# A linear-attention and mixture-of-experts kernel: block 0's x in halves, and another order in the drain behind the last block

## The chip, the cores and the metric

The kernel runs on one core of a Trainium2 chip, in one launch. Its time is the device time of an execution in microseconds (us). Engines are named as in the profile: PE is TensorE (matmuls), PEld its weight loads, DVE is VectorE, ACT is ScalarE, POOL is GpSimd, SP is SyncE, which here only issues DMAs.

## What is computed

```
phi(x): a = S1 x, b = S2 x (8 values each); phi = outer(a, b), 64 values
kv = phi(k)^T v,  z = sum phi(k);   attn = phi(q) kv / (phi(q) z + 1e-6)        # 4 batches, 4 heads, 1088 tokens, dim 32
x  = attn as 4352 tokens x 128
xn = x / sqrt(mean(x*x) + 1e-6) * rms_g
y  = (silu(xn w_gate) * (xn w_val)) w_out                                        # hidden size 1536
logits = y phi2                                                                  # 32 slots, 4 for each of 8 experts
D = softmax of logits over tokens (each slot);  slot_input = D^T y               # 32 x 128
slot_out[e] = relu(slot_input[e] w1[e]) w2[e]                                    # hidden size 1024, 8 experts
C = softmax of logits over slots (each token);  out = C slot_out                 # 4352 x 128
```

All inputs and outputs are float32. The three large products of the second layer are made from a rounded high part and a low part of each operand (`xh`, `xl`, `wgh`, `wgl`, ...), with three matmuls for each product.

## The kernel before

The program is written engine by engine; every engine has its own list of instructions in program order, and semaphores join them. The order is by hand, there is no planner.

**Blocks.** The tokens are split into nine blocks: 0 to 7 of 512 tokens (two for each batch) and block 8 (`NB`) of the 256 tokens that remain. A block is run by `whole_block` in 12 steps `c`, one for each 128 hidden columns: `gate_value` (6 matmuls of 512 columns, L1012), then SiLU on ACT, product `hid` on DVE (L764), rounding `hh` on ACT (L527), rest `hl` on DVE (L770), and `output` (3 matmuls, L1025). The gate matmuls run `LAG` = 3 steps ahead of the output matmuls. Between these steps the attention and the normalisation of the next block are made.

**The head.** Before block 0 there is no earlier block to hide behind. Its x goes through `attention` (DVE, L715), `squares` (ACT, L492), `mean_square` (DVE, L722 and L724), `inverse_rms` (POOL, L424), `normalised` (DVE, L731), `normalised_T` (PE, L981, into `bank_a`), `scaled_T` (ACT, L496, `xh`) and `split_x` (DVE, L737, `xl`). Among these ACT rounds thirds of the three weight matrices (`split_hi`, L568) and POOL forms what rounding leaves (`split_lo`, L419). Piece x of matrix n is n = 0 gate, 1 val, 2 out. In program order ACT has val 0, out 0, val 1, squares, out 1 and so on, and POOL has gate 0, gate 1, val 0, out 0, val 1, `inverse_rms(0)`. `keep_clock(n)` is n matmuls of the identity with itself whose result nobody reads. SP and ACT issue the input loads; ACT's list has the last 64 keys of every batch (`k_rem`, rows of 256 bytes, L474).

**The drain.** A product of slots needs the maximum over all tokens of each slot's logit. `cmax_a` is the maximum over blocks 0 to 6 (28 tiles of 128 tokens, `NA`); in block 8 their logits get that maximum subtracted (L836), and ACT takes the exponential afterwards (L595). Behind block 8, PE makes its logits, DVE the maximum over the last six tiles (L865, L868), PE transposes it, DVE reduces it (`cm_all`, L870), PE spreads it, DVE subtracts it (L875), ACT takes the exponential (L600). `dispatch` sums exp(logit) x y in four groups of 32 partitions, the first 28 tiles in one bank, the last six in another. ACT rescales the first (`part_a`, L606), DVE adds them (L879), PE sums the four groups (`rep`), DVE divides (L882 to L886), PE transposes (L1161), ACT copies (`slotT`, L609). Then come the experts: `hidden` in four calls of 4 matmuls (n is the half of the experts, hf the half of the 1024 columns), Relu on ACT (L618), four transposes for each call (`hidden_T`, L1175), copies of each expert's own rows into the zeroed `hTz` (DVE, L893), and `slots_out`. Last, `s_out` is copied (L621), spread by `rep` and copied (`so4`, L623), and nine groups of output matmuls with the transposed combine weights `combT` follow; DVE and ACT scale them (L907, L628), SP stores them (L395, L399).

## Time and profile before

| | |
|---|---|
| time, median of 3 runs | 309.48 us (308.49 to 310.48) |
| the profiled execution | 311.83 us |
| its span, first to last instruction | 309.7 us |
| mean granted TensorE clock | 0.981 of full |
| PE busy | 295.4 us (95%), 2599 matmul instructions |
| PEld, DVE, ACT, POOL busy | 240.7, 224.2, 165.9, 29.7 us |
| chain that ended last | PE 87%, DMA 4%, DVE 3%, SP's queue 2%; its largest line, L915 (matmuls), 82% |

The table says how full the engines are over the whole span. The chain follows the work back from the last instruction to what released each piece, so it says which of that work set the end. The granted clock has two levels, 1.00 (2.4 GHz) and 0.50 (1.2 GHz); a stretch with a number between them has both.

### The profile page before, as it was taken

The numbers are of one execution on the slowest core, as the hardware profiler recorded it, in microseconds if no ns is written. First come the engines' busy times: TensorE is split into PE (matmuls) and PEld (weight loads), VectorE is DVE, ScalarE is ACT, GpSimd is POOL, SyncE is SP. The second block draws the span as 40 slices with busy tenths as digits, with TensorE's granted clock in tenths as the row PEclk, the third lists the DMA queues.
The fourth block names the chain that finished last, engine by engine and source line by source line (L and its number), as shares of the span: only waits on it lengthen the run. The fifth ranks groups of instructions, "written<-read, shape, count | busy, mean of one in ns | idle before, by whom it ended". The sixth has DMA issues, their size and how long they took to land.

```text
span 309.7 us, 6608 instructions
## 1 busy us (share of the span) xinstructions
PE 295.4 (95%) x2599; PEld 240.7 (78%) x2599; DVE 224.2 (72%) x438; ACT 165.9 (54%) x313; POOL 29.7 (10%) x49
## 2 busy tenths in 40 slices
PE   7769999999999999999999999999999999998985
PEld 7668788888888888888888778887888788896363
DVE  4733979786789688959877797687678758875144
ACT  1643566634755557355665564466545555557412
POOL 1356001000100010002500100020010001000000
PEclk9997999999999999999999999999999999999995
DMA  7999200000001200100030013999100100110007
GB/s 186 354 228 203 70 3 1 2 0 2 0 11 25 71 0 11 28 1 2 13 69 23 0 17 69 418 358 271 26 3 0 25 11 0 17 21 0 4 4 286
DMA packets 34864, 21.94 MB, mean 71 GB/s; under 512 B 19473, under 2 KB 31506, under 8 KB 34834
## 3 DMA queue, kind: packets, MB, share of 16 engines
q1 hardware_dynamic: 34162, 21.13, 24.9%
q10 hardware_dynamic: 672, 0.39, 0.6%
q8 instruction: 20, 0.33, 0.4%
q14 instruction: 10, 0.08, 0.1%
HBM read 17.45 MB, written 2.23 MB: 64 GB/s over the span
## 4 chain that ended last, share of the span: by engine, by line
PE 87%; DMA 4%; DVE 3%; SPq 2%; issue 1%; POOL 1%; ACT 1%; DVEq 0%; ACTq 0%; POOLq 0%
PE bank L915 82%; DMA area<-in_moe_w_out 4%; PE bank L954 2%; PE bank L981 1%; SPq L333 1%; PE bank L1175 1%; POOL wol L419 0%; DVE hid L764 0%; POOL wvl L419 0%; DVE area L907 0%; DVE cmax_a L821 0%; POOL rstd L424 0%; DVE hl L770 0%; SPq L339 0%; DVE area L731 0%
## 5 line engine op out<-in xcount | busy, mean ns | idle before, releaser
L764 DVE TENSOR_TENSOR hid<-bank,silu 128x512 f32<-128x512 f32 (+1 forms) x108 | 71.0, 657 | 49.9 <-PE bank L915 27.0
L519 ACT ACTIVATE silu<-bank 128x512 f32<-128x512 f32 (+1 forms) x108 | 61.9, 573 | 69.5 <-PE bank L915 68.5
L770 DVE TENSOR_TENSOR hl<-hid,hh 128x512 fp32r<-128x512 f32 (+1 forms) x108 | 70.2, 650 | 0.1
L527 ACT ACTIVATE hh<-hid 128x512 fp32r<-128x512 f32 (+1 forms) x108 | 64.9, 601 | 3.5 <-DVE hid L764 3.5
L915 PE MATMUL bank<-hh,woh 128*128 128x512 f32 (+1 forms) x108 | 43.4, 402 | 0.4 <-DVE hl L770 0.4
L915 PE MATMUL bank<-xh,wgh 128*128 128x512 f32 (+1 forms) x108 | 43.1, 399 | 0.5 <-DVE hid L764 0.5
L915 PE MATMUL bank<-xh,wgl 128*128 128x512 f32 (+1 forms) x108 | 41.3, 382 | 0.0
L915 PE MATMUL bank<-xh,wvh 128*128 128x512 f32 (+1 forms) x108 | 41.3, 382 | 0.0
L915 PE MATMUL bank<-xh,wvl 128*128 128x512 f32 (+1 forms) x108 | 41.1, 380 | 0.0
L915 PE MATMUL bank<-hh,wol 128*128 128x512 f32 (+1 forms) x108 | 41.1, 380 | 0.0
L915 PE MATMUL bank<-xl,wgh 128*128 128x512 f32 (+1 forms) x108 | 41.1, 380 | 0.0
L915 PE MATMUL bank<-hl,woh 128*128 128x512 f32 (+1 forms) x108 | 40.9, 379 | 0.0
L915 PE MATMUL bank<-xl,wvh 128*128 128x512 f32 (+1 forms) x108 | 40.8, 378 | 0.0
L424 POOL TENSOR_TENSOR rstd<-msq,mhalf 128x4 f32<-128x4 f32 (+1 forms) x9 | 8.8, 976 | 192.0 <-DVE msq L724 191.9
L915 PEld LDWEIGHTS bank<-hh,woh 128*128 128x128 f32 x108 | 20.3, 188 | 5.0 <-DVE hl L770 0.6
L915 PEld LDWEIGHTS bank<-xh,wgh 128*128 128x128 f32 x108 | 20.5, 189 | 4.3 <-DVE hid L764 0.9
L915 PEld LDWEIGHTS bank<-xl,wvh 128*128 128x128 f32 x108 | 20.4, 189 | 4.1
L915 PEld LDWEIGHTS bank<-xh,wgl 128*128 128x128 f32 x108 | 20.4, 189 | 4.1
L915 PEld LDWEIGHTS bank<-xh,wvl 128*128 128x128 f32 x108 | 20.3, 188 | 4.1
L915 PEld LDWEIGHTS bank<-hh,wol 128*128 128x128 f32 x108 | 20.3, 188 | 4.1
L915 PEld LDWEIGHTS bank<-xh,wvh 128*128 128x128 f32 x108 | 20.4, 189 | 3.9
L915 PEld LDWEIGHTS bank<-xl,wgh 128*128 128x128 f32 x108 | 20.5, 190 | 3.5
(134 smaller groups left out, 352.1 us busy)
## 6 DMA issues: line engine op xcount, KB each, us to landing
area<-in_moe_w SPq DMA_DIRECT2D x1, 4096.0 KB, 12.7
area<-in_moe_w SPq DMA_DIRECT2D x8, 512.0 KB, 7.0
q_in<-in_q SPq DMA_DIRECT2D x16, 128.0 KB, 2.7
y_nat<-in_v SPq DMA_DIRECT2D x4, 512.0 KB, 7.6
out<-area SPq DMA_DIRECT2D x8, 256.0 KB, 2.2
area<-in_k SPq DMA_DIRECT2D x14, 128.0 KB, 7.2
y_nat<-area SPq DMA_DIRECT2D x112, 16.0 KB, 1.8
area<-in_moe_w_gate SPq DMA_DIRECT2D x1, 768.0 KB, 6.2
```

The costliest lines, as they stand in the source:

```text
L333: sp.dma_start(dst[h * D:(h + 1) * D, :], src[h, 0:TM * P, :].rearrange("(u n) d -> u (n d)", u=D))\
L424: pool.tensor_tensor(rstd[:, 0:nt], msq[:, 0:nt], mhalf[:, 0:nt], ALU.pow).then_inc(s_rstd_ready, 1)
L519: act.activation(silu[n][:, 0:w], gate_b[n][:, 0:w], ACT.Silu).then_inc(s_silu_ready, 1)
L527: act.activation(hh[m % NH][:, 0:w], hid[m % 2][:, 0:w], ACT.Copy).then_inc(s_hh_ready, 1)
L764: dve.tensor_tensor(hid[n][:, 0:w], val_b[n][:, 0:w], silu[n][:, 0:w], ALU.mult).then_inc(s_hid_ready, 1)
L770: dve.tensor_tensor(hl[m % NH][:, 0:w], hid[m % 2][:, 0:w], hh[m % NH][:, 0:w].bitcast(F32), ALU.subtract).then_inc(s_hl_ready, 1)
L915: return pe.matmul(o, l, r, start=start, stop=stop)
L954: ins = pe.transpose((bank_a, bank_c)[hp][:, t * P:(t + 1) * P], qp[:, t, hp * P:(hp + 1) * P], ident[:, :])
L981: ins = pe.transpose(bank_a[:, t * P:(t + 1) * P], x_n[:, t, :], ident[:, :])
L1175: ins = pe.transpose(hT_b[2 * n + hf][:, c * P:(c + 1) * P], h_slots[:, n, (4 * hf + c) * P:(4 * hf + c + 1) * P], ident[:, :])
```

## The change

Two edits were joined.

In the head, block 0's squares, sums, normalisation, transposes, `xh` and `xl` are made in two halves of 256 tokens (`HH` = 2 tiles); the second half's transposes go to `bank_c`. On ACT the squares come before the first piece of w_out, on POOL `inverse_rms(0)` comes before every piece but gate 0, gate 1 and val 0. `k_rem` of batches 1 to 3 is loaded by SP behind batch 1's values. `keep_clock` counts are 16 and 5 in place of 18 and 6.

In the drain, `NA` is now 32 tiles: block 7's logits, their maximum and the combine transposes of blocks 0 to 7 are made inside block 8 (PE steps 1, 4, 6, 10 and 11; DVE steps 2, 3, 5, 7 and 8). Behind it block 8's logits are made transposed (`lT_b`, slots on partitions), so that the maximum, the exponential (with `accum_out` for the sum) and the shift are per partition. The slot inputs of block 8 and of the rest are summed in one accumulation, already transposed (`slotT_b`); division by the sum waits until `so4`. `slotZ` holds each expert's four slots with zeros around, so that `hidden` needs two calls of 8 matmuls, `hidden_T` 8 transposes and DVE 4 copies. Combine exponentials are taken after the transposes. `keep_clock(1)` and `keep_clock(2)` stand around the `rep` matmul.

```diff
@@ SP and ACT: loads
+                    for h in range(H):
+                        sp.dma_start(k_rem[h * D:(h + 1) * D, 1:B, :], ...).then_inc(s_krem_loaded, 16)
                     sp.dma_start(phi_sb[:, :], phi).then_inc(s_phi_loaded, 16)
-                act.dma_start(k_rem[h * D:(h + 1) * D, :, :], ...
+                act.dma_start(k_rem[h * D:(h + 1) * D, 0, :], ...
@@ POOL
             split_lo(1, 0, wvh, wvl, s_wv_hi, s_wv_lo)
+            inverse_rms(0)
+
+            pool.wait_ge(s_xn_ready, 1)
             split_lo(2, 0, woh, wol, s_wo_hi, s_wo_lo)
             split_lo(1, 1, wvh, wvl, s_wv_hi, s_wv_lo)
-            inverse_rms(0)
-
-            pool.wait_ge(s_xn_ready, 1)
@@ ACT: squares, scaled_T (and likewise DVE: mean_square, normalised, split_x; PE: normalised_T)
+                if jn == 0:
+                    act.wait_ge(s_x_ready, 1)
+                    act.activation(x_sq[:, 0:HH, :], x_at[:, 0:HH, :], ACT.Square).then_inc(s_xsq0_ready, 1)
+                    act.wait_ge(s_x_ready, 2)
+                    act.activation(x_sq[:, HH:HT, :], x_at[:, HH:HT, :], ACT.Square).then_inc(s_xsq_ready, 1)
+                    return
...
@@ DVE behind block 8
+            dve.wait_ge(s_lT_ps, 1)
+            dve.tensor_reduce(cm_b[:, :], lT_b[0:NS, 0:WR], axis=AX.X, op=ALU.max).then_inc(s_cmb_ready, 1)
+            dve.wait_ge(s_cmb_ready, 1)
+            dve.tensor_scalar(cm_neg[:, :], cm_b[:, :], cm_a[:, 0:1], -1.0, ALU.max, ALU.mult).then_inc(s_cmneg_ready, 1)
+            dve.wait_ge(s_cmneg_ready, 1)
+            dve.tensor_tensor(cm_diff[:, :], cm_a[:, :], cm_neg[:, :], ALU.add).then_inc(s_cmdiff_ready, 1)
+            dve.wait_ge(s_disp_ps, 1)
+            dve.tensor_copy(disp[:, NA:NT, :], ...).then_inc(s_disp_ready, 1)
             logits(NB)
...
+            dve.wait_ge(s_slotT_ps, 1)
+            dve.tensor_copy(slotZ.rearrange("p (e c) -> p e c", c=ZP)[:, :, 0:SPE], ...).then_inc(s_slotT_ready, 1)
@@ ACT behind block 8
-            act.activation(disp[:, 0:NA, :], disp[:, 0:NA, :], ACT.Exp).then_inc(s_dispa_ready, 1)
+            for x in range(2):
+                tiles = slice(x * NA // 2, (x + 1) * NA // 2)
+                act.wait_ge(s_dshifta_ready, x + 1)
+                act.activation(disp[:, tiles, :], disp[:, tiles, :], ACT.Exp).then_inc(s_dispa_ready, 1)
+            act.wait_ge(s_cmneg_ready, 1)
+            act.activation(dispT[:, :], lT_b[0:NS, 0:WR], ACT.Exp, bias=cm_neg[:, 0:1], accum_out=sum_b[:, :])
@@ PE in block 8
+                    if last and c >= C - 2:
+                        pe.wait_ge(s_cshift_ready, NB)
+                        pe.wait_ge(s_hid_ready, C * NB + c + 1)
+                        comb_transposes(4 * (c - C + 2), 4 * (c - C + 2) + 4)
@@ PE behind block 8
+            for t in range(NA, NT):
+                mm(slotT_b[:, 0:NS], y_nat[:, t, 0:P], disp[:, t, :], t == NA, False)
+            pe.wait_ge(s_parta_ready, 1)
+            mm(slotT_b[:, 0:NS], part_a[:, 0:P], rep[:, 0:NS], False, True).then_inc(s_slotT_ps, 1)
...
-            hidden(0, 0)
-            hidden(0, 1)
-            hidden_T(0, 0)
-            hidden(1, 0)
...
+            hidden(0)
+            hidden(1)
+            pe.wait_ge(s_ssum_ready, 1)
+            hidden_T(0)
+            hidden_T(1)
             pe.wait_ge(s_w2_loaded, 16 * E)
+            slots_out(0)
+            slots_out(1).then_inc(s_so_ps, 1)
```

How it moves instructions at three places. First ACT in the head, from the first rounding of w_gate to the first SiLU: before,

```order
L568 ACTIVATE wgh<-area 128x512 x2
L486 ACTIVATE area<-bank 128x512 x2
L568 ACTIVATE wvh<-area 128x512
L568 ACTIVATE woh<-area 128x512
L568 ACTIVATE wvh<-area 128x512
L492 ACTIVATE area<-area 128x512
L568 ACTIVATE woh<-area 128x512
L568 ACTIVATE wgh<-area 128x512
L568 ACTIVATE wvh<-area 128x512
L568 ACTIVATE woh<-area 128x512
L496 ACTIVATE xh<-bank,g_col 128x512
L519 ACTIVATE silu<-bank 128x512 x2
```

and with the change:

```order
L594 ACTIVATE wgh<-area 128x512 x2
L498 ACTIVATE area<-bank 128x512 x2
L594 ACTIVATE wvh<-area 128x512 x2
L505 ACTIVATE area<-area 128x256
L507 ACTIVATE area<-area 128x256
L594 ACTIVATE woh<-area 128x512 x2
L594 ACTIVATE wgh<-area 128x512
L594 ACTIVATE wvh<-area 128x512
L594 ACTIVATE woh<-area 128x512
L515 ACTIVATE xh<-bank,g_col 128x256
L518 ACTIVATE xh<-bank,g_col 128x256
L545 ACTIVATE silu<-bank 128x512 x2
```

The squares (area from area) stood behind the first `woh` piece; now they stand ahead of every `woh` piece, in two halves, and `xh` comes in two halves too.

Second POOL in the head, before and then with the change; `rstd` is `inverse_rms(0)`:

```order
L419 TENSOR_TENSOR wgl<-area,wgh 128x512 x2
L419 TENSOR_TENSOR wvl<-area,wvh 128x512
L419 TENSOR_TENSOR wol<-area,woh 128x512
L419 TENSOR_TENSOR wvl<-area,wvh 128x512
L424 TENSOR_TENSOR rstd<-msq,mhalf 128x4
L419 TENSOR_TENSOR wol<-area,woh 128x512
```

```order
L430 TENSOR_TENSOR wgl<-area,wgh 128x512 x2
L430 TENSOR_TENSOR wvl<-area,wvh 128x512
L435 TENSOR_TENSOR rstd<-msq,mhalf 128x4
L430 TENSOR_TENSOR wol<-area,woh 128x512
L430 TENSOR_TENSOR wvl<-area,wvh 128x512
L430 TENSOR_TENSOR wol<-area,woh 128x512
```

Two pieces of `split_lo` that stood ahead of `rstd` now stand behind it.

Third PE behind block 8, from the logits to the first `hidden` matmul, before:

```order
L915 MATMUL bank<-phi_sb,yT 32x32 x8
L1003 MATMUL bank<-ident,yT 128x128 x2
L915 MATMUL bank<-y_nat,area 32x129 x8
L1137 MATMUL bank<-ident,cmax 32x128
L915 MATMUL bank<-y_nat,area 32x129 x8
L915 MATMUL bank<-cdiag,ones 128x32
L915 MATMUL bank<-cm_diff,rep 128x1
L915 MATMUL bank<-y_nat,area 32x129 x18
L1150 MATMUL bank<-ident,comb 128x128 x4
L915 MATMUL bank<-part,rep 128x129
L1150 MATMUL bank<-ident,comb 128x128 x5
L1161 MATMUL bank<-ident,slot_n 128x128
```

and with the change:

```order
L956 MATMUL bank<-yT,phi_sb 32x256
L1042 MATMUL bank<-ident,yT 128x128 x2
L956 MATMUL bank<-y_nat,area 32x129 x16
L956 MATMUL bank<-cm_diff,rep 128x1
L956 MATMUL bank<-y_nat,area 32x129 x16
L1199 MATMUL bank<-ident,dispT 128x32 x2
L956 MATMUL bank<-phi_sb,yT 32x32 x8
L956 MATMUL bank<-area,y_nat 128x32 x2
L956 MATMUL bank<-rep,part_a 128x32
L956 MATMUL bank<-part_a,rep 128x1
L956 MATMUL bank<-sum_b,rep 128x1
L956 MATMUL bank<-area,slotZ 32x512 x16
```

The maximum's transposes and spreading, the combine transposes, the `part` matmul and the transposing of `slot_n` are gone from between; `dispatch` has 32 matmuls in place of 34, and block 8's share goes through `slotT_b` as two matmuls of 32 columns. The `hidden` matmuls now stand in one run of 16 before the first transposes.

## Rows read from the trace of the kernel before

**Rows 1.** The chain of waits up to block 0: start us, length us, what.
```profile
6.91 11.75 DMA area<-in_moe_w_out
...
18.69 0.64 ACT woh L568
...
19.39 1.28 POOL wol L419
...
22.00 1.03 POOL rstd L424
```

**Rows 2.** The timeline, 16 to 31 us: start, length, engine, line, operation.
```profile
16.65 4.29 PE L915 MATMUL bank<-ident 128*128 128x128 f32 x36
...
17.31 0.75 DVE L715 TENSOR_TENSOR area<-bank,rden 128x256 f32<-128x256 f32 x2
...
19.74 0.61 ACT L492 ACTIVATE area<-area 128x512 f32<-128x512 f32 x1
...
21.11 0.81 DVE L724 TENSOR_SCALAR msq<-ssq 128x4 f32<-128x4 f32 x1
...
24.56 0.69 ACT L496 ACTIVATE xh<-bank,g_col 128x512 fp32r<-128x512 f32 x1 [2.12 <-PE bank L981]
...
26.27 0.77 PE L915 MATMUL bank<-xh,wgh 128*128 128x512 f32 x1
...
28.63 0.39 PE L915 MATMUL bank<-xh,wgh 128*128 128x512 f32 x1
...
30.01 0.39 PE L915 MATMUL bank<-xh,wgh 128*128 128x512 f32 x1
```

**Rows 3.** Stretches: length, busy us (instructions) per engine, granted clock, DMA share, GB/s.
```profile
25.00:26.00 1.00, 1.00 (x7) 1.00 (x7) 0.72 (x1) 0.25 (x1) 1.00 (x2) 0.50 1.04 234
...
300.00:301.00 1.00, 0.52 (x16) 0.33 (x12) 0.57 (x2) 0.58 (x2) 0.00 (x0) 1.00 0.00 0
...
301.00:302.00 1.00, 0.95 (x16) 0.86 (x16) 0.70 (x2) 0.30 (x2) 0.00 (x0) 0.63 0.10 39
```

**Rows 4.** The timeline of VectorE, 256 to 262 us.
```profile
257.06 0.41 DVE L722 TENSOR_REDUCE ssq<-area 128x2 f32<-128x256 f32 x1
...
257.51 0.17 DVE L724 TENSOR_SCALAR msq<-ssq 128x2 f32<-128x2 f32 x1
...
261.28 0.48 DVE L737 SCALAR_TENSOR_TENSOR xl<-bank,g_col,xh 128x256 fp32r<-128x256 f32 x1
```

**Rows 5.** The timeline by engine, 271 to 299 us.
```profile
271.36 0.29 PEld L915 LDWEIGHTS bank<-cdiag_a,ones 32*128 32x128 f32 x2 [0.28 <-issue]
...
280.00 0.39 PE L915 MATMUL bank<-hh,woh 128*128 128x256 f32 x1 [0.36 <-DVE hl L770]
...
281.14 0.42 DVE L859 COPY yT<-bank 128x256 f32<-128x256 f32 x1 [0.71 <-PE bank L915]
...
282.29 0.65 PE L915 MATMUL bank<-y_nat,area 128*32 128x129 f32 x16
...
286.48 0.49 PE L915 MATMUL bank<-part,rep 128*128 128x129 f32 x2
...
288.51 1.92 PE L915 MATMUL bank<-area,slotT 128*32 128x512 f32 x16 [0.38 <-ACT slotT L609]
...
290.37 0.66 PE L1175 MATMUL bank<-ident,area 128*128 128x128 f32 x4
...
291.06 0.42 DVE L893 COPY hTz<-bank 128x16 f32<-128x16 f32 x4 [3.31 <-PE bank L1175]
...
297.03 1.27 DVE L898 TENSOR_REDUCE csum<-comb 128x34 f32<-128x1088 f32 x1
...
298.61 0.28 ACT L621 ACTIVATE s_out<-bank 128x128 f32<-128x128 f32 x1 [4.34 <-PE bank L915]
```

**Rows 6.** The chain of waits in the output phase.
```profile
301.05 0.67 PE bank L915 x8
...
306.05 0.56 DVE area L907
```

More of the change, by code:

```diff
@@ L138, in fused_attention_moe @@
         crec = sb("crec", [P, NT])
-        part_a, part = sb("part_a", [P, P + 1]), sb("part", [P, P + 1])
+        part_a = sb("part_a", [P, P + 1])
         srec = sb("srec", [P, 2])
-        slot_n = sb("slot_n", [P, P])
-        slotT = sb("slotT", [P, NS])
+        ZP = NS + SPE
+        slotZ = sb("slotZ", [P, E * ZP])
         psum = ctx.enter_context(nc.psum_tensor("bank", [P, 8 * 512], F32))
@@ L605, in _, with combine_T @@
             act.wait_ge(s_parta_ps, 1)
-            act.activation(part_a[:, :], part_b[0][:, 0:P + 1], ACT.Copy, scale=scale_a[:, 0:1]).then_inc(s_parta_ready, 1)
-            act.wait_ge(s_slotT_ps, 1)
-            act.activation(slotT[:, :], slotT_b[:, 0:NS], ACT.Copy).then_inc(s_slotT_ready, 1)
-            for n in range(3):
+            act.activation(part_a[:, :], part_b[:, 0:P + 1], ACT.Copy, scale=scale_a[:, 0:1]).then_inc(s_parta_ready, 1)
+            def combine_T(n):
                 act.wait_ge(s_combT_ps, n + 1)
@@ L978, in normalised_T @@
             def normalised_T(jn):
+                if jn == 0:
+                    for h, ready, done in ((0, s_xn0_ready, s_xT0_ps), (1, s_xn_ready, s_xT_ps)):
+                        pe.wait_ge(ready, 1)
+                        for t in range(HH):
+                            ins = pe.transpose((bank_a, bank_c)[h][:, t * P:(t + 1) * P], x_n[:, HH * h + t, :], ident[:, :])
+                        ins.then_inc(done, 1)
+                    return
                 pe.wait_ge(s_xn_ready, jn + 1)
@@ L1092, in whole_block @@
                         finish(j - 1)
-                    if last and c == 0:
+                    if last and c == 1:
+                        pe.wait_ge(s_yT_ready, NB)
+                        pe.wait_ge(s_x_ready, 2 * (NB + 1))
+                        logits(NB - 1)
+                    if last and c == 4:
                         pe.wait_ge(s_cmaxa_ready, 1)
@@ L1119, in _, with dispatch @@
             whole_block(NB, 0, B, last=True)
[L1120 to L1123 removed]
+            def dispatch(t0, t1):
                 for t in range(t0, t1):
                     c = t % 4
[L1127 to L1132 removed]
@@ L1144, in _ @@
+            dispatch(NA // 2, NA).then_inc(s_parta_ps, 1)
+            pe.wait_ge(s_dispT_ready, 1)
+            for t in range(NT - NA):
+                ins = pe.transpose(lT_b[:, WR + t * NS:WR + (t + 1) * NS], dispT[:, t * P:(t + 1) * P], ident[0:NS, 0:NS])
+            ins.then_inc(s_disp_ps, 1)
+            pe.wait_ge(s_logit_ready, NB)
+            logits(NB)
             pe.wait_ge(s_disp_ready, 1)
             pe.wait_ge(s_y_ready, NB + 1 - NY)
-            dispatch(NA, NT, part_b[1], NA, NT).then_inc(s_part_ps, 1)
@@ L1158, in _ @@
-            mm(slot_b[:, 0:P + 1], rep[:, :], part[:, :]).then_inc(s_rep_ps, 1)
-            comb_transposes(4, NTP // 4)
-            pe.wait_ge(s_slotn_ready, 1)
-            pe.transpose(slotT_b[:, 0:P], slot_n[:, :], ident[:, :]).then_inc(s_slotT_ps, 1)
-            def hidden(n, hf):
-                for x in range(4):
-                    ins = mm(h_b[2 * n + hf][NS * x:NS * (x + 1), :], slotT[:, :],
-                             w1_sb[:, 4 * n + x, hf * 512:hf * 512 + 512])
-                ins.then_inc(s_h_ps, 1)
@@ L1182, in slots_out, with hidden @@
+            pe.wait_ge(s_parta_ready, 1)
+            mm(slotT_b[:, 0:NS], part_a[:, 0:P], rep[:, 0:NS], False, True).then_inc(s_slotT_ps, 1)
+            mm(bank_a[:, 2 * P + 1:2 * P + 2], rep[:, :], part_a[:, P:P + 1], True, False)
+            mm(bank_a[:, 2 * P + 1:2 * P + 2], rep[0:NS, :], sum_b[:, :], False, True).then_inc(s_sum_ps, 1)
+            def hidden(hf):
+                for n in range(2):
                     for x in range(4):
                         e = 4 * n + x
-                        ins = mm(so_b[NS * x:NS * (x + 1), 0:P], hTz[:, e, fc, :], w2_sb[:, e, fc, :],
-                                 start=(n == 0 and fc == 0), stop=(n == 1 and fc == FC - 1))
+                        ins = mm(h_b[hf][NS * x:NS * (x + 1), :], slotZ[:, e * NS:(e + 1) * NS],
+                                 w1_sb[:, e, hf * 512:hf * 512 + 512], start=n == 0, stop=n == 1)
+                ins.then_inc(s_h_ps, 1)
@@ new lines, in hidden_T, with slots_out @@
+            def hidden_T(hf):
+                pe.wait_ge(s_h_ready, hf + 1)
+                for c in range(4):
+                    ins = pe.transpose(hT_b[hf][:, c * P:(c + 1) * P],
+                                       h_slots[:, (4 * hf + c) * P:(4 * hf + c + 1) * P], ident[:, :])
+                ins.then_inc(s_hT_ps, 1)
+            def slots_out(hf):
+                pe.wait_ge(s_hT_ready, hf + 1)
+                for fc in range(4 * hf, 4 * hf + 4):
+                    for n in range(2):
+                        for x in range(4):
+                            e = 4 * n + x
+                            ins = mm(so_b[NS * x:NS * (x + 1), 0:P], hTz[:, e, fc, :], w2_sb[:, e, fc, :],
+                                     start=(n == 0 and fc == 0), stop=(n == 1 and fc == FC - 1))
```

241 lines of the change are left out of this document (114 added, 127 removed).

## The prediction

> **What bounds the kernel now.** I read the page first: PE is busy 95% of the span, and 87% of the chain lies on it. Time can come only from the places where the chain leaves PE, so I read the chain in order of time. Its largest line by far, 82%, is the matmuls of L915. It leaves PE for long at two places.
>
> The head, until 26.27 us. The chain there is not attention: it goes from the landing of w_out (18.66) through the rounding of its first piece on ACT and `split_lo` on POOL, which is busy until 21.9, and only then come `rstd`, x_n, the transposes, `xh`, `xl` [rows 1]. The reason is program order. x was ready at 17.31 + 0.75 = 18.06, but its squares started at 19.74, behind `woh`, and the sum's scaling took 0.81 us and ended only when POOL's piece did [rows 2]; at 2 tiles it takes 0.17 [rows 4]. The identity matmuls that bridge the wait end at 20.94, PE then stands almost 3 us, until the transposes just ahead of `xh` at 24.56, and the granted clock is 0.50 at 25 to 26 us [rows 2, 3]. Six matmuls take 28.63 - 26.27 = 2.36 us there, the next six 1.38 [rows 2].
>
> The drain, from 281.14. There small steps alternate between engines: 7.37 us from block 8's `yT` to the first `hidden` matmul (288.51), then 10.10 us to `s_out` (298.61), then the output phase [rows 5, 6].
>
> **The head, part by part.** With squares ahead of `woh` and `rstd` ahead of the pieces, the chain starts from x at 18.06. Half-size operations I price by the 256-column rows: 0.41 for a reduction, 0.48 for `xl` [rows 4]. Second half of the squares until 18.5, its sum 18.95, scaling 19.15 (0.17, as POOL is idle), `rstd` 1.03 [rows 1] 20.2, x_n in two halves (0.41 to 0.48 each, like the others [rows 4], the second starting early) 21.0. The first half's transposes run beside the second half's x_n; they end near 21.1, the others at 21.45.
>
> ACT is then late next: behind the squares stand five roundings, the first of which needs w_out at 18.66. From 18.69 to 19.74 two of them started [rows 1, 2], so 0.52 apart; five end at 18.69 + 4 x 0.52 + 0.63 = 21.4. `xh` in halves, 0.45 apart, until 22.3 (0.69 for the whole, [rows 2]), `xl`'s second half 0.48, and the first gate matmul at 22.85. The 16 identity matmuls end at 16.65 + 16 x 4.29 / 18 = 20.5 and the 5 others near 22.7, so they don't hold it up. That is 3.4 us sooner. Moving three quarters of `k_rem` behind the weights lets v and w_out land a little earlier; I have no row for how much, bounds 0 and 0.5 (a gain as long as ACT or the values are late), and take 0.1. Head: **-3.5** (bounds -3.0, if each handover costs 0.1 more, and -3.9).
>
> PE's gaps are now 0.2 to 0.3 us where one of almost 3 was, so the clock should stay at 1.00: 2.36 - 1.38 = **-1.0** (bounds 0 and -1.0). PE bounds blocks 0 to 7, so both pass on whole. The later loads have time: they are needed in block 0's steps 2, 3 and 8. The delayed `split_lo` pieces run while PE makes the first three gate steps, 1.38 each, at 1.28 for a piece [rows 1, 2]; the piece of w_out that the first output needs is ready at 22.4, before the first gate matmul.
>
> **The drain, part by part.** Inside block 8, PE gets block 7's logits at another step (no cost) and 8 combine transposes (1.2 us) between outputs 9, 10 and 11, where it waited 0.36 for `hl` anyway [rows 5]. DVE's two subtractions (0.7 each) now stand ahead of the last `hl`, which comes 0.4 later. Against this PE no longer waits 0.28 for the early maximum [rows 5]. Sum: block 8's end **+0.3** (0 to +0.8, if none of the transposes fits into a wait).
>
> From `yT` to `hidden`, times from `yT`'s start: copy 0.42; the transposed logits, 256 columns in two passes, 0.75 with their way out (129 columns take 0.49 [rows 5]); maximum of 32x256, 0.41 as any reduction of 256 [rows 4], near 1.65. Its followers (`cm_neg`, the exponential) run beside PE, which goes on with 2 transposes and 32 dispatch matmuls: 8 take 0.65 [rows 5], so 2.4, and with the small matmul between PE is through at 3.85. Then dispT's transposes with their way out and DVE's copy, 0.65, until 4.5; `part_a` is ready at the same time; the summing matmuls and their way out 0.45; DVE has the logits of block 8 in front of `slotZ` until 5.0; copy 0.22 and handover. `hidden` starts at 5.25 instead of 7.37: **-2.1** (bounds -2.6 and 0, the latter if the small handovers add up as before).
>
> The experts: 16 `hidden` matmuls cost what they did (1.92 for each 8 [rows 5]), 64 slot matmuls likewise, which is 10.10 less 3.85 and four stretches of transposes of 0.6 [rows 5]: 3.85. Those stretches fall to two; one is followed by a wait of 0.1 to 0.2 on Relu, the copies of `hTz` (0.42 for four [rows 5], now two at a time) on the way. 3.85 + 0.6 + 0.15 + 0.6 + 0.05 + 3.85 = 9.15 against 10.10: **-0.95** (-0.6 to -1.2).
>
> The output phase: the clock falls in 301 to 302, after stretches half idle [rows 3]. A PE step and a DVE step alternate, 0.67 and 0.57 [rows 6]; at full rate the former is some 0.1 shorter. Filling the two waits ahead of it may keep the clock up for a few of the nine steps: **-0.25** (0 to -0.8, all nine). `csum`, the combine exponentials and block 8's shift have 2 us or more beside the experts' matmuls: nothing; without that cover the sum alone would cost 1.27 [rows 5].
>
> Sum: -3.5 - 1.0 + 0.3 - 2.1 - 0.95 - 0.25 = **-7.5**. The profiled execution took 311.83, so it would be 304.3; the median of the three runs is 309.48, which gives **302.0**. Both differ from each other by 2.35, and I take the median as the base.
>
> **Where a page speaks against it.** The clock was still 1.00 at 300 to 301 us [rows 3], though transposes made much of PE's work between waits. The Trainium skill, TensorE: Matmul & The Clock Gate, Part 4: PE-mode transpose, says that transposes do not count as busy for the clock. The change puts eight of them in one run between `hidden` and `slots_out`; by that rule the first slot matmuls could run at 1.2 GHz. Its price is in the third rival.
>
> **The rivals.** *The drain gives nothing before `hidden`.* The new path has as many handovers as the old: `part_a` waits for ACT, DVE makes block 8's logits between two urgent copies, `hl` is late. For: 7.37 us for little work shows that handovers rule there. Against: the transposed form removes four of them. Then -4.5 + 0.3 - 0.95 = -5.15: 304.3. Chance 0.2.
>
> *The clock dips in the head all the same*, because the first matmuls come after two short gaps. -6.5: 303.0. Chance 0.08.
>
> *The clock falls in the drain*, before `dispatch`, since PE has gaps of 0.5 us at `yT` and at `slotZ`, and thin work between. 2.4 + 3.85 + 3.85 = 10.1 us of PE work then take twice as long, the gains of clock in head and output phase are gone: -3.5 + 0.3 - 2.1 - 0.95 + 10.1 = +3.9: 313.4, slower. It decides from 6.2 us of slowed work on. In a smaller form, it falls at the transposes ahead of `slots_out` and only the slot matmuls double: -7.5 + 0.25 + 3.85 = -3.4, 306.1. Against: today's gap of 0.38 at `slotT` [rows 5], and a like one at `yT`, left it at 1.00 up to 301 [rows 3]. Chances 0.04 and, for the smaller, 0.02.
>
> *The loads hold the head.* If the values or w_out land a microsecond later than today, half of the head's 4.5 is lost: 304.2. Chance 0.05. The forecast has the rest, 0.61.
>
> **How the numbers follow.** All terms at their best bound give -9.5, 300.0; all at their worst -2.8, 306.7, and neither is likely to meet in one run. The first, second and fourth rival lie at 303.0 to 304.3 with the same spread of a microsecond around them. Range 300.3 to 305.3, with less than 2 in 10 outside. Within 1% of before, which is about what a measurement of this kernel can tell from no change, is 306.4 to 312.6. Only many worst bounds at once, or a rival with them, reach it. Faster by over 1%: 0.92; within: 0.04; slower by over 1%: 0.04.
>
> **What would show it.** Head: the first gate matmul near 22.8, and the first six in 1.4 us; squares starting before 18.1; the scaling near 0.2 us; `xh` starting right behind the last rounding. Drain: `slotZ` copied 5 us after `yT`; `s_out` 9.2 us after the first `hidden`; granted clock 1.00 until then. Wrong would be: a wait of block 0 for a load, `xh` waiting for transposes instead of ACT, the last output waiting over 1 us for `hl`, or a granted clock below 1.00 between 275 and 290 us.

## The result, and the profile after

The changed kernel takes 306.2 us (median of 4, 305.58 to 308.99), the kernel before 309.98 beside it (4, 308.49 to 310.84): ratio 0.9888, 95% interval 0.9844 to 0.9932. It is faster by 1.1%, half of what was forecast: 302.0 us, range 300.3 to 305.3, missed by 4.2. The profiled execution of the change took 306.57 (span 304.3), that of the kernel before 311.83 (span 309.7), 5.3 less where the sum said 7.5. Of the miss of 4.2, 2.2 is therefore in the terms and 2.0 in the base. One of the change's four executions, 308.99, has a mean granted clock of 0.986 instead of 0.990 to 0.994; it was not profiled, so what made it long is open.

By stages, each time from the span's start:

| | before | before, run again | after | forecast |
|---|---|---|---|---|
| x ready | 18.06 | 17.93 | 17.52 | 18.06 |
| first gate matmul | 26.27 | 25.46 | 23.41 | 22.8 |
| first six matmuls | 2.36 | 1.50 | 1.50 | 1.4 |
| features of block 1 (first transposes) | 38.38 | 36.70 | 34.95 | 33.9 |
| block 8, `cmax_a` to `yT` | 15.78 | 15.79 | 16.52 | 16.1 |
| `yT` to `hidden` | 7.37 | 7.36 | 5.73 | 5.25 |
| `hidden` to `s_out` | 10.10 | 10.10 | 9.41 | 9.15 |
| `s_out` to the end | 11.09 | 10.64 | 10.77 | 10.85 |

The chain of waits of the changed kernel in the head, beside [rows 1]: start us, length us, what.

```profile
6.87 12.48 DMA area<-in_moe_w_out
19.37 1.15 ACT woh L594 x2
...
21.57 0.52 ACT woh L594
22.09 0.37 ACT xh L515
...
22.48 0.48 DVE xl L773
22.96 0.40 DVE xl L776
...
23.41 5.79 PE bank L956 x24
...
29.32 0.68 DVE hl L813
```

POOL and `rstd` are gone from it. It still begins with the landing of w_out, and now goes through ScalarE's five roundings to `xh`. The timeline of the changed kernel, 16 to 30 us, ACT, then DVE, POOL and PE, beside [rows 2]:

```profile
17.22 0.42 ACT L505 ACTIVATE area<-area 128x256 f32<-128x256 f32 x1 [1.24 <-DVE area L745]
...
19.37 1.15 ACT L594 ACTIVATE woh<-area 128x512 fp32r<-128x512 f32 x2 [1.40 <-DMA area<-in_moe_w_out]
...
18.46 0.17 DVE L758 TENSOR_SCALAR msq<-ssq 128x4 f32<-128x4 f32 x1
...
26.55 0.69 DVE L807 TENSOR_TENSOR hid<-bank,silu 128x512 f32<-128x512 f32 x1 [0.68 <-PE bank L956]
27.16 1.52 DVE L813 TENSOR_TENSOR hl<-hid,hh 128x512 fp32r<-128x512 f32 x1
...
29.32 0.68 DVE L813 TENSOR_TENSOR hl<-hid,hh 128x512 fp32r<-128x512 f32 x1
...
26.82 1.31 POOL L430 TENSOR_TENSOR wol<-area,woh 128x512 fp32r<-128x512 f32 x1
...
23.41 0.50 PE L956 MATMUL bank<-xh,wgh 128*128 128x512 f32 x1 [1.27 <-DVE xl L776]
```

The scaling takes 0.17 where it took 0.81. ACT had finished the squares by 17.97 and then waited 1.40 us for w_out, so x's rounding waited too. And there is a row that the prediction did not have: the first `hl` takes 1.52 us, the next one 0.68. Stretches of the changed kernel, columns as in [rows 3]:

```profile
25.00:26.00 1.00, 1.00 (x6) 0.83 (x5) 0.69 (x1) 0.23 (x2) 1.00 (x2) 1.00 1.12 236
290.00:291.00 1.00, 1.00 (x48) 1.00 (x40) 0.00 (x0) 0.00 (x0) 0.00 (x0) 1.00 0.00 0
300.00:301.00 1.00, 0.01 (x2) 0.00 (x0) 0.63 (x2) 0.37 (x1) 0.00 (x0) 0.81 0.46 146
```

The clock is 1.00 under block 0's gates and under the slot matmuls (290 to 291), right behind eight transposes in one run; it falls at the very end. The drain, by engine, beside [rows 5]:

```profile
278.39 0.42 DVE L909 COPY yT<-bank 128x256 f32<-128x256 f32 x1 [0.71 <-PE bank L956]
...
279.86 1.09 PE L956 MATMUL bank<-y_nat,area 128*32 128x129 f32 x32
...
282.54 0.23 DVE L917 COPY area<-bank 128x64 f32<-128x64 f32 x1 [2.12 <-PE bank L1199]
...
282.82 0.63 PE L956 MATMUL bank<-area,y_nat 128*128 128x32 f32 x4
283.29 0.39 PE L956 MATMUL bank<-rep,part_a 128*128 128x32 f32 x2
283.51 0.36 PE L956 MATMUL bank<-part_a,rep 128*128 128x1 f32 x2
...
283.78 0.19 DVE L922 COPY slotZ<-bank 128x32 f32<-128x32 f32 x1 [0.59 <-PE bank L956]
...
284.12 3.64 PE L956 MATMUL bank<-area,slotZ 128*32 128x512 f32 x32
287.69 1.44 PE L1224 MATMUL bank<-ident,area 128*128 128x128 f32 x8
289.06 3.03 PE L956 MATMUL bank<-area,hTz 128*32 128x128 f32 x101
292.43 1.06 PE L956 MATMUL bank<-area,hTz 128*32 128x128 f32 x27 [0.34 <-issue]
```

Up to 282.77 every step stands where it was forecast: the logits' maximum done 1.62 us after `yT` starts (forecast 1.65), dispatch through at 3.8 (3.85; its second half 281.18 to 282.20), DVE's copy done at 4.38 (4.5). Then the summing matmuls: from 282.82 to `slotZ`'s start at 283.78 are 0.96 us, where 0.45 were forecast; the profile counts two instructions for each of them (x4 for two, x2 for one). In the slot matmuls stands a gap of 0.34 behind the 101st.

### The profile page after: what moved, and what is told of

Its sections match the earlier page's. It is cut to its first block, busy times and chain, and to the rows that moved or that the text cites. A ratio compares the mean times of both kernels' runs of the same rounds, so it can differ in the third digit from the quotient of the medians.

```text
span 304.3 us, 6596 instructions
## 1 busy us (share of the span) xinstructions
PE 291.7 (96%) x2595; PEld 238.0 (78%) x2595; DVE 223.0 (73%) x428; ACT 165.7 (54%) x314; POOL 29.8 (10%) x50
## 3 DMA queue, kind: packets, MB, share of 16 engines
HBM read 17.45 MB, written 2.23 MB: 65 GB/s over the span
## 4 chain that ended last, share of the span: by engine, by line
PE 85%; DVE 4%; DMA 4%; SPq 2%; ACT 2%; issue 2%; DVEq 0%; ACTq 0%
PE bank L956 81%; DMA area<-in_moe_w_out 4%; PE bank L995 2%; PE bank L1029 1%; DVE hl L813 1%; SPq L341 1%; DVE area L948 1%; DVE hid L807 1%; ACT woh L594 1%; DVE area L725 0%; PE bank L1107 0%; DVE cmax_a L864 0%; DVE area L699 0%; PE bank L1042 0%; SPq L347 0%
## 5 line engine op out<-in xcount | busy, mean ns | idle before, releaser
L813 DVE TENSOR_TENSOR hl<-hid,hh 128x512 fp32r<-128x512 f32 (+1 forms) x108 | 71.1, 658 | 0.0
```

Source lines behind the costliest of these rows:

```text
L813: dve.tensor_tensor(hl[m % NH][:, 0:w], hid[m % 2][:, 0:w], hh[m % NH][:, 0:w].bitcast(F32), ALU.subtract).then_inc(s_hl_ready, 1)
```

## The experiments

Sixteen runs, all read on the stage times above. "Gate" is the first gate matmul.

**The kernel before, again.** No edit.

> The kernel before, unchanged. Theory A (its profiled execution of 311.83 us was an untypical one, whose head waited long for w_out): the head differs from execution to execution; here w_out lands one to two us before 18.7, block 0's squares start early and the first gate matmul stands at 24 to 25.5 instead of 26.27, span near 307.5. Theory B (the head is always as in that trace, the 2 us lie in the drain or outside the span): first gate matmul at 26.0 to 26.5 again.

310.52 us (median of 10) against 309.92 (22), ratio 1.0019 (0.9995 to 1.0043). Its profiled execution, 309.73, has no fall of the clock in the head; windows as in [rows 3]:

```profile
25.00:26.00 1.00, 0.72 (x4) 0.48 (x3) 0.41 (x1) 0.00 (x0) 1.00 (x2) 1.00 1.01 245
```

Yet PE had stood 2.40 us before its normalised transposes. The times lie in two groups, five at 309.3 to 310.1 and five at 310.9 to 311.7. The five longer ones have a mean granted clock of 0.981 to 0.986, the five shorter ones 0.986 to 0.992. So the trace on which the prediction rests (311.83, clock 0.981) was one of the longer kind: against this second trace the change saves 3.2 us, not 5.3. Theory A had the gate and the span right, but w_out landed only 0.6 earlier (18.04). Of the 2.1 us between the two spans, 0.8 stand ahead of the gate, 0.9 in the six matmuls and 0.4 behind `s_out`.

**The head's half alone; the drain's half alone.** The diff cut into its two parts:

```diff
-(e2) NA = NB * HT, lT_b, slotT_b, dispT, slotZ, comb_transposes in block 8, ...
-(e3) HH halves, squares ahead of woh, inverse_rms(0) ahead of the pieces, k_rem on SP
```

> The kernel before with the edits of the head alone (halves, order on ACT and POOL, k_rem, keep_clock 16 and 5). From the two traces: features_T of block 1 ends 3.4 us earlier than in the first trace of before. If that trace was typical, the time is 3.4 us (1.1%) under before; if theory A holds, only 1.5 to 2 us (0.5 to 0.6%). Either way the first hl on VectorE takes over 1.2 us in place of 0.68 if a piece of split_lo on GpSimd runs at that time.

> The kernel before with the edits of the drain alone. From the two traces: +0.74 in block 8, -1.64 from yT to hidden, -0.69 in the experts, -0.33 in the output phase, together -1.9 us (0.6%) under before, whatever the head does. If the drain's gain were conditional on the head, it would differ by over 0.5 us from that.

Head: 307.9 us, ratio 0.9923 (0.9893 to 0.9953). Drain: 308.44, ratio 0.996 (0.9928 to 0.9992). Together -0.77 and -0.40%, the whole -1.12%: the halves add up within their intervals. The head's 2.0 us is what theory A gave (1.5 to 2), the drain's 1.5 is near the 1.9 expected. With the head alone the gate stands at 23.61 and the stages of the drain are those of the kernel before. With the drain alone block 8 takes 16.52, `yT` to `hidden` 5.73, `hidden` to `s_out` 8.70, so these are the drain's own terms. Its execution has the slow clock in the head (six matmuls 2.23 us), with the old head's order. PE in the head, in the second trace of before, then with the drain alone; the x12 row is `keep_clock(6)`:

```profile
23.18 0.66 PE L981 MATMUL bank<-ident,area 128*128 128x128 f32 x4 [2.40 <-DVE area L731]
23.67 1.50 PE L915 MATMUL bank<-ident 128*128 128x128 f32 x12
```

```profile
23.70 0.66 PE L986 MATMUL bank<-ident,area 128*128 128x128 f32 x4 [2.38 <-DVE area L738]
24.19 2.46 PE L920 MATMUL bank<-ident 128*128 128x128 f32 x12
```

PE stood 2.40 us in the one and 2.38 in the other, behind the same bridge of 4.29 us; the clock stayed at 1.00 in the first and fell between 24 and 25 us in the second. So the length of the idle stretch alone does not say whether the clock falls.

**`k_rem` back on ScalarE's queue, whole.** Was it the moved load that let w_out land late?

```diff
-for h: sp.dma_start(k_rem[h, 1:B], ...)      # behind batch 1's values
+act.dma_start(k_rem[h, :], ...)              # as before
```

> The changed kernel with k_rem of all batches back on ScalarE's list. If moving k_rem made the weights land later (12.05 to 12.8 for w_gate, 18.66 to 19.35 for w_out), they land 0.7 us earlier here and the first gate matmul comes 0.5 to 0.7 us sooner (22.8). If that difference was chance between executions, the first gate matmul stands within 0.3 us of the changed kernel's, or later by what v lands later.

306.05 us, ratio 0.9876 (0.9841 to 0.9911), as the changed kernel. w_out lands at 18.43, 0.9 sooner than in the changed kernel (19.35), and the gate comes at 22.77, as the first theory had it. But e15 below keeps the moved load, and there w_out lands at 17.47. Over the traces in which w_out's load is not delayed, it lands at 16.91 to 18.66 with the old placement (6 traces, median 18.2) and at 17.26 to 20.06 with the new (10, median 18.6): if the moved load costs anything, it is less than this scatter.

**A POOL piece earlier; POOL's pieces in halves.**

```diff
-(e5) inverse_rms(0); ...; split_lo(2, 0); split_lo(1, 1); ...
+(e5) split_lo(1, 1); inverse_rms(0); ...; split_lo(2, 0); ...
-(e6) pool.tensor_tensor(lo[:, piece], ...)          # 128x512
+(e6) for y in range(2): pool.tensor_tensor(lo[:, half], ...)   # 128x256
```

> The changed kernel with one GpSimd piece (w_val's second, split_lo) put back ahead of inverse_rms(0), into the 1.4 us in which GpSimd idled there. Port theory (VectorE's hl, two SBUF inputs, waits until the running GpSimd instruction ends): GpSimd is done 1.25 us sooner, at 26.9, before the first hl at 27.2, so that hl takes 0.68 instead of 1.52 and features_T of block 1 starts 0.3 us nearer to the first gate matmul (11.2 instead of 11.54 behind it). Rival theory (the 1.5 us hl is a wait for ScalarE's hh, or DMA traffic on SBUF): it stays near 1.5.

> The changed kernel with each split_lo of GpSimd as two instructions of 256 columns in place of one of 512. Port theory: hl waits at most for one instruction of some 0.65 us, so it ends by 28.2 and takes under 1.3 us; if what blocks is GpSimd's being busy at all and not the single instruction, it still ends only with the last one, 1.5 us.

e5: 305.8 us, ratio 0.9835 (0.9774 to 0.9895); in its profiled execution w_out landed early (17.26), `woh` started right behind the squares (17.54), x was at 17.18 and the gate at 21.88. POOL was through at 26.54, as wanted, but the first `hl` stood at 25.63, met the last piece and took 1.45: POOL's pieces follow x_n, `hl` follows the gate, and here the gate was 1.5 sooner. e6, one execution: 304.82. The timeline of e6, DVE and POOL, 26 to 30 us:

```profile
26.67 0.94 DVE L814 TENSOR_TENSOR hl<-hid,hh 128x512 fp32r<-128x512 f32 x1
...
28.25 1.21 DVE L814 TENSOR_TENSOR hl<-hid,hh 128x512 fp32r<-128x512 f32 x1
...
28.17 1.89 POOL L430 TENSOR_TENSOR wol<-area,woh 128x256 fp32r<-128x256 f32 x2
```

A half piece makes one `hl` wait less, but now two wait, and two POOL halves take 1.89 beside them (the last two pieces both) instead of 1.43. From the gate to block 1's transposes it is 11.51 us, in the changed kernel 11.54: halving moved the cost, it did not remove it. What settles the first theory is the end of `hl`. In all thirteen traces with the head's edits, and in both `hl` of e6, every `hl` that starts beside a POOL instruction ends 0.54 to 0.56 us behind that instruction's end, whether it then takes 0.94 or 1.52 us; the five traces with the old head have no such meeting, and `hl` takes 0.68.

**w_out's high part behind x's rounding.**

```diff
-split_hi(2,0) split_hi(2,1) wg3 wv3 split_hi(2,2)  xh  silu
+wg3 wv3  xh  split_hi(2,0) split_hi(2,1) split_hi(2,2)  silu      # ScalarE
+split_lo(1,1) ahead of inverse_rms(0); split_lo(2,0..2) last        # GpSimd
```

> The changed kernel with the three roundings of w_out on ScalarE behind xh instead of ahead of it, and w_val's second split_lo ahead of rstd. If ScalarE's wait for w_out (landed at 19.35) sets the head, xh starts right behind the transposes (20.8 instead of 22.0) and the first gate matmul stands near 22.3 instead of 23.4, hl takes 0.7; together 1.3 to 1.5 us (0.4 to 0.5%) under the changed kernel. If the transposes or the identity matmuls set it, the gate matmul stands at 23 or later. If block 0's VectorE chain is the bound, as the 25 to 35 us of the krem run suggest, under half of the gain is left at the end of features_T.

305.59 us, ratio 0.9825 (0.9768 to 0.9883). Gate 21.79, 4.69 behind x (17.10) instead of 5.89. The first `hl` takes 1.47 and not 0.7, since the last w_out pieces now lie beside it. The time alone does not show the gain: e5 and e8 beside it, with w_out in front, take 305.8 and 305.34, and w_out landed early in this trace (17.35). Two kernels then made w_out late on purpose, in both orders.

```diff
-sp.dma_start(w_raw[2], w_out)       # behind w_val
+sp.dma_start(w_raw[2], w_out)       # behind batch 1's k
```

> The changed kernel with w_out's load issued behind the k loads of the next batch. Theory (ScalarE waits for w_out ahead of x's last roundings, and that sets the first gate): w_out's high part starts some 1 to 2.5 us later than the 18.5 to 19.4 us it has in the changed kernel, and the first gate matmul is later by the same (24.5 to 26 us), time 1 to 2.5 us over the changed kernel. Rival (x's own chain on VectorE and GpSimd sets it): first gate unchanged at 22.8 to 23.4 us.

> e7 (w_out's high part rounded behind x's first six rounded pieces) with w_out's load as late as in e12. Theory (only ScalarE's place in line tied the gates to w_out): first gate matmul at 21.8 to 22.6 us, 2 us ahead of e12's 24.53, and about 304.5 us. Rival (the loads behind each other delay the values too, and x with them): first gate at 23.5 us or more; or the first output matmul waits for w_out's high part, which would show as a wait of over 0.5 us in block 0's first steps.

e12: 307.38 us, ratio 0.992 (0.9879 to 0.9961). e13, one execution: 305.94. ACT in e12, then ACT and PE in e13:

```profile
20.50 1.15 ACT L594 ACTIVATE woh<-area 128x512 fp32r<-128x512 f32 x2 [2.61 <-DMA area<-in_moe_w_out]
```

```profile
21.65 0.47 ACT L515 ACTIVATE xh<-bank,g_col 128x256 fp32r<-128x256 f32 x1 [1.94 <-PE bank L1024]
...
22.38 1.67 ACT L594 ACTIVATE woh<-area 128x512 fp32r<-128x512 f32 x3
...
21.11 0.77 PE L1024 MATMUL bank<-ident,area 128*128 128x128 f32 x4 [0.48 <-DVE area L766]
...
23.09 0.51 PE L956 MATMUL bank<-xh,wgh 128*128 128x512 f32 x1
```

With w_out in front x's rounding waits for it; with x in front ACT stands idle 1.94 us for the transposes, and the gate depends on x alone. No output matmul of block 0 waits for w_out in e13. Its gate is 0.5 later than expected because x was (18.22), and because w_val landed at 16.23 (13.4 to 14.8 where w_out's load is not moved), so that POOL's two pieces ahead of `rstd` ended only at 19.47 and `rstd` began 0.17 later behind x. All thirteen traces with the head's edits fall under one rule, the later of two: x + 4.7 (4.87 in e13), and first `woh` + 4.03 if w_out stands in front. In e4 and e15 the first `woh` begins right behind the squares, without a wait for the load, so the last column says nothing of it there.

| | x | `woh` | gate | behind x | behind `woh` |
|---|---|---|---|---|---|
| after | 17.52 | 19.37 | 23.41 | 5.89 | 4.04 |
| e2 | 17.65 | 19.58 | 23.61 | 5.96 | 4.03 |
| e12 | 17.44 | 20.50 | 24.53 | 7.09 | 4.03 |
| e4 | 18.08 | 18.45 | 22.77 | 4.69 | 4.32 |
| e15 | 17.78 | 18.14 | 22.47 | 4.69 | 4.33 |
| e7 | 17.10 | behind | 21.79 | 4.69 | |
| e13 | 18.22 | behind | 23.09 | 4.87 | |

**Block 8: the subtractions or the transposes?** e8 moved both, e15 the transposes alone, e14 starts from e9 (e7 and e8 joined) and takes all transposes out.

```diff
-(e8, e9, e14) if last and c in (7, 8):    # DVE's two subtractions
+(e8, e9, e14) if last and c in (6, 7):
-(e8, e9, e15) comb_transposes(4, 8) ahead of output 11
+(e8, e9, e15) comb_transposes(4, 8) behind output 11
+(e14)         comb_transposes(0, 8) behind output 11
```

> The changed kernel with VectorE's two subtractions in block 8 one step earlier (6 and 7, where VectorE idled 1.2 us) and the second four combine transposes behind the last output instead of ahead of it. If the subtractions ahead of hl make block 8 0.73 us longer, maximum to yT falls from 16.52 to 16.1 or less; if the combine transposes themselves cost it, it falls by 0.44 and comes back as a later start of the lT matmul; if it is the early maximum's steps 1 to 4, it stays at 16.5.

> e9 with all eight combine transposes behind block 8's last output instead of four between outputs 10 and 11. Theory (TensorE has no free time in block 8, each four transposes cost their 0.6 us there less a wait they fill): maximum to yT falls from 16.16 us to 15.5 to 15.8; yT to hidden grows by 0.1 to 0.6, since four transposes more stand ahead of the transposed logits (the first four fit into the wait of 0.7 for the copy of yT). Rival (VectorE's subtractions make block 8 longer): maximum to yT stays at 16.1 to 16.2.

> The changed kernel with the last four combine transposes behind block 8's last output; the subtractions stay in VectorE's steps 7 and 8. Theory (transposes on TensorE): maximum to yT 16.1 to 16.2 us as in e8 and e9, against 16.52. Rival (the subtractions ahead of the last hl): stays at 16.45 or more, TensorE waiting 0.3 to 0.6 us for the last hl.

| | subtractions | transposes inside | block 8 | `yT` to `hidden` |
|---|---|---|---|---|
| after | 7, 8 | 8 | 16.52 | 5.73 |
| e15 | 7, 8 | 4 | 16.51 | 5.66 |
| e8, e9 | 6, 7 | 4 | 16.16 | 5.66 |
| e14 | 6, 7 | none | 16.16 | 5.95 |

The output matmul of PE that waits for `hl`, output 11 in e15, then output 10 in e14:

```profile
277.15 0.39 PE L956 MATMUL bank<-hh,woh 128*128 128x256 f32 x1 [0.31 <-DVE hl L813]
```

```profile
275.95 0.39 PE L955 MATMUL bank<-hh,woh 128*128 128x256 f32 x1 [0.47 <-DVE hl L812]
```

What transposes leave, PE spends waiting for `hl`; they cost nothing in the block. The theory that I put forward for e14 and e15 is wrong, the rival right: e8 and e15 differ in the subtractions' steps alone, and that costs 0.35. By its place it is the second one, which stands between the last `hid` and the last `hl` (e5 and e6, without an edit here, have 16.45 instead of 16.52, so 0.07 of it can be scatter). e8 took 305.34 us (ratio 0.9826, 0.9761 to 0.9891), e14 304.89 and e15 305.21 in one execution each. The other 0.37 of the 0.73 is not taken apart. Rows of e14 against the second trace of before show pieces of it: from `cmax_a` on, output 9 starts at 13.94 instead of 13.78, and output 10, for which PE waits on `hl`, at 14.92 instead of 14.65.

**e7 and e8 joined, and the last stores.** e10 is e9 with block 8's two stores issued by ScalarE.

```diff
+(e10) act.wait_ge(s_o_ready, n + 1); act.dma_start(out[...], o_sb[...])   # 2 stores
-(e10) sp.dma_start(out[...], o_sb[...])
```

> The changed kernel with k_rem where it was in the kernel before, w_out's high part rounded behind x's first six rounded pieces, and the two subtractions and four of the combine transposes of the last block placed as in e8. Theory (ACT's wait for w_out holds x's rounding; the drain's extra VectorE work stands in block 8's chain): first gate matmul at 21.8 to 22.8 us, maximum to yT 16.2 us, yT to hidden 5.66, hidden to last weights 8.70, last weights to the end 10.8; 304.2 to 305.0 us, ratio to the kernel before 0.978 to 0.984. Rival (the gains do not add because the output phase is bound by stores): same first gate, but the tail grows over 11.2 us and the time stays at 305.5 or more.

(That text is wrong in one point: e9's `k_rem` is loaded as in the changed kernel.)

> e9 with the two stores of block 8's outputs issued by ScalarE's queue instead of SyncE's. Theory (the end of the kernel is set by SyncE issuing ten stores one behind another): last weights to the end falls from 10.8 us to 10.0 to 10.4, time 0.4 to 0.8 us under e9. Rival (the stores' transfers themselves are the bound): still 10.7 to 10.9, time as e9 within 0.2 us.

e9: 304.61 us (6, 304.06 to 304.81), ratio 0.9802 (0.9766 to 0.9839), with every stage where it was expected (gate 22.58). It is the lowest ratio of all; the changed kernel's, measured at another time, is 0.9888 (0.9844 to 0.9932), so e9 is faster than it by some 0.9%. e10: 305.13, ratio 0.9832 (0.9791 to 0.9873), not clear of e9. Issues on SP in e9, then ScalarE's and SP's in e10:

```profile
294.12 2.01 SPq L405 DMA_DIRECT2D out<-area  x4
...
297.78 2.04 SPq L405 DMA_DIRECT2D out<-area  x4
```

```profile
296.16 1.36 ACTq L660 DMA_DIRECT2D out<-area  x2
297.56 0.63 ACT L654 ACTIVATE area<-bank,crec 128x128 f32<-128x128 f32 x2 [2.18 <-DVE area L948]
...
298.08 1.24 PE L956 MATMUL bank<-so,area 32*128 32x128 f32 x16 [1.39 <-ACT area L654]
```

The two issues hold ScalarE for 1.36 us, its copies come late, and PE waits 1.39: `s_out` to the end 11.17 instead of 10.77. So e10 made another wait and does not decide. The other traces do: in the twelve with the new drain and all stores on SP, the last DVE operation ends 7.10 to 7.72 us behind `s_out`, but the issues of SP's last four stores begin 6.22 or 6.23 and end 8.25 to 8.27 behind it in each of them (297.78 to 299.82 in e9, with `s_out` at 291.56), and the kernel ends 10.76 to 10.81 behind it. With the five traces of the old drain, where the last issue ends at 8.11 to 8.55, the end lies 2.50 to 2.55 behind the last issue in all seventeen. So the end follows SP's issues and not the last scaling, as the theory had it; what fewer or other issues would give no run shows.

**Longer bridges in the head of the kernel before.**

```diff
-keep_clock(18, bank[2])
+keep_clock(28, bank[2])      # e11
+keep_clock(23, bank[2])      # e16
```

> The kernel before with 28 filling matmuls instead of 18 ahead of block 0's gates, so that TensorE idles less before the first gate matmul. Theory (in about half of the executions of the kernel before the clock falls to 1.2 GHz under block 0's gates, and those make up the upper group of times near 311.3 us): the six gate matmuls 1.50 us, granted clock 1.00 there, no execution in the upper group, median 0.5 to 1.0 us under the kernel before's. Rival (the two groups come from when w_out and x land): both groups stay, ratio 0.999 to 1.001. If the filling matmuls reach past x's landing, the first gate comes later instead and it is slower by that much.

> The kernel before with 23 bridging matmuls instead of 18. Theory (TensorE's 2.4 to 3 us of idleness ahead of the normalised transposes brings the clock down in some executions, and a bridge that ends 1.2 us later prevents it without holding the transposes): six gate matmuls 1.50 us, first gate at 25.5 to 26.3, median 0.3 to 0.9 us under the kernel before's, fewer than 3 of 12 executions over 310.9. Rival (the slower executions come from an early fall of the clock, at 12 to 15 us as e11's trace showed it, or from late loads): a third to a half of the executions over 310.9, ratio 0.998 to 1.002.

e11: 310.34 us, ratio 1.001 (0.9982 to 1.0039), and five of 12 executions over 310.9. Its profiled one, 311.86, had the clock at 1.00 under the gates but low earlier, and its bridge reached past x_n:

```profile
12.00:13.00 1.00, 1.00 (x26) 1.00 (x22) 1.00 (x1) 0.80 (x2) 0.08 (x1) 0.50 0.94 373
...
25.00:26.00 1.00, 1.00 (x12) 1.00 (x10) 0.00 (x0) 0.45 (x1) 1.00 (x2) 1.00 1.28 269
```

```profile
18.50 6.52 PE L915 MATMUL bank<-ident 128*128 128x128 f32 x56
24.86 0.60 PE L981 MATMUL bank<-ident,area 128*128 128x128 f32 x4
```

x_n was done at 23.33 and its transposes began at 24.86: 28 is too long in this execution, in which x came late (19.93), behind the low clock. The theory, no execution in the upper group, is refuted for 28. e16: 309.6 us (12, 308.66 to 310.47), ratio 0.9981 (0.9961 to 1.0), and none of its 12 executions over 310.9, where the kernel before, over all its executions beside the experiments, had 21 of 68, and 5 of 17 beside this one. PE in e16:

```profile
16.55 5.40 PE L915 MATMUL bank<-ident 128*128 128x128 f32 x46
22.07 0.66 PE L981 MATMUL bank<-ident,area 128*128 128x128 f32 x4
...
24.35 0.50 PE L915 MATMUL bank<-xh,wgh 128*128 128x512 f32 x1 [0.28 <-DVE xl L737]
```

A bridge 1.2 us longer thus seems to take away the group of longer times, for some 0.5 us of the median, which fits a clock that falls in the head in about a third of the executions of the kernel before. It is not more than that: 0 of 12 against 5 of 17 can still be chance, the interval of the ratio reaches 1.0, and w_out landed earliest of all in this trace (16.91), so that PE stood only 0.1 us ahead of the transposes. That the fall in the head is the whole difference between the two groups of times is not shown either: e11's fall at 12 to 15 us is another one.

## Why the prediction was wrong, step by step

The step that failed first is the base; then come the sizes of four terms. Against the trace that they were read from, the terms missed by 1.07 us up to block 1's transposes (-3.43 instead of -4.5: 0.64 at the gate, 0.14 in the six matmuls, 0.29 behind them), by 0.44 in block 8, 0.46 from `yT` to `hidden`, and 0.26 in the experts.

**The base.** "I take the median as the base" for terms measured on another kind of execution. The profiled one lay 2.35 over the median, and I saw it, but took from the median what that execution paid and many others did not: the fall of the clock (1.0 by the terms, 2.36 against 1.50 for six matmuls), w_out's late landing (18.66 against 18.04) and the clock's earlier fall at the end (11.09 against 10.64). Against the second trace of before the head's gain to block 1 is 36.70 - 34.95 = 1.75, not 4.5. Of the 4.2 missed, 2.0 come from here: the change's profiled execution lies 0.4 over its median, that of before 2.35. The mechanism of the clock was right, the term was counted where it did not apply.

**The head, -3.5.** The chain named there is what the runs show: ScalarE's roundings last, `woh` + 4.03 where the forecast had 22.85 - 18.69 = 4.16. (x's own chain it did not price up to the gate; it had the last transposes end 3.4 us behind x, and they end 3.5 behind it.) What was wrong is one input: w_out at 18.69, as in one trace. e4 happens to have the forecast's inputs, x at 18.08 and `woh` at 18.45, and its gate is at 22.77 where 22.85 was forecast. But the landing scatters, and in the changed kernel's profiled execution `woh` began at 19.37, hence 23.41 and -2.86. "ACT is then late next" was right, but it should have been priced as a wait on a load with a spread instead of as fixed. "The loads hold the head" (0.05) was half true there: not block 0 but ScalarE's place in line tied them to the gates, and e7 undoes it.

**A term missing.** "The delayed `split_lo` pieces run while PE makes the first three gate steps": they cost POOL nothing, but they cost VectorE. From the gate to block 1's transposes the second trace of before takes 11.24 us, the changed kernel 11.54 with one `hl` held up, and e4, e8 and e15 11.9 with two. So a gate 0.64 sooner (e4) brings block 1 only 0.30 sooner. The first `hl` starts at 27.16 and ends at 28.68, 0.55 behind POOL's piece (28.13), while `hid`, one of whose inputs is a bank, takes its usual 0.69 beside POOL. The Trainium skill, SBUF — State Buffer, "SBUF: two separate sides", says that a VectorE operation with two SBUF inputs and a GpSimd one that reads SBUF exclude each other: whichever starts first holds their shared ports for the whole instruction. The trace agrees, 1.52 against 0.68 for `hl` and no change for `hid`. The other way round shows too: in e4, e8 and e15 the last piece starts while `hl` still runs and takes 1.76 to 1.78 instead of 1.31. The prediction had seen the same sign in the scaling, 0.81 us until POOL's piece ended, and used it there alone. Moved work has to be laid over every neighbour, not over PE alone.

**The clock stays up, -1.0.** Right in mechanism: 1.49 to 1.51 for six matmuls in all thirteen traces with the head's edits, none of which is of the change's long execution.

**Block 8, +0.3.** Measured +0.73. The subtractions were named ("comes 0.4 later") and are 0.35. I had set against them 0.28 that PE no longer waits for the early maximum. That is a misreading of [rows 5]: the 0.28 is idle time of the weight loads (PEld), marked "issue", and PE's own matmuls stand only 0.10 us there, 271.29 to 271.39. There was no 0.28 to win.

**`yT` to `hidden`, -2.1.** Measured -1.64, and the step is the one already shown, 0.96 instead of 0.45 for the summing matmuls. The rival that the drain gives nothing there is refuted.

**The experts, -0.95.** The terms written there add up to 9.10, not 9.15. Measured -0.69 in the changed kernel and -1.4 in nine of the thirteen traces with the drain's edits; 9.13 to 9.42 us instead of 8.70 in the other four, each with a gap behind the 101st slot matmul (0.34 in after, 0.35 in e12, 0.07 in e4 and e13) that the nine don't have. The gap is not all of it (0.71 in after), and what it is stays open.

**The output phase, -0.25.** `s_out` to the end is 10.64 to 10.69 with the old drain (without the early fall of the clock) and 10.76 to 10.81 in every kernel with the new but e10: nothing gained. In the changed kernel the clock did stay up longer, until 7.1 us behind `s_out` instead of 4.9 in the second trace of before, but SP's store issues set the end, not the matmuls. SP's first one begins 2.56 us behind `s_out` with the new drain and 2.41 with the old, which is about the 0.13 by which it is later.

In the drain the clock never fell before `s_out` in any trace, so the slower rival did not come; eight transposes in a row (1.44 us) left it at 1.00.

## What to carry to other kernels

Take a second profile of the same kernel before pricing terms, and ask of each term whether both executions pay it; subtract from the execution that shows it. Where an in-order engine waits for a load whose landing scatters, put nothing urgent behind that wait. When GpSimd work is moved, look which VectorE operations with two SBUF inputs it will then lie beside. And at an end made of stores, look first whether the last compute or the issuing queue moves the end.
